# A DeltaNet and MoE kernel: the opening reordered, low weight parts on GpSimd, contiguous sums in the triangular solve

## The reference, cut to what matters

```python
# attention: delta rule, B=4, H=8, S=768, D=48
k_n = k / (norm(k) + 1e-6)
for t in range(S):
    y[t] = q[t] @ state
    state = state + beta[t] * outer(k_n[t], v[t] - k_n[t] @ state)
x = y of all heads, as (3072, 384)
# first expert layer: no nonlinearity between w3 and w_out
x = ((x @ w1) * (x @ w2)) @ w3 @ w_out          # 384 -> 1024 -> 1024 -> 384
# second layer: SoLU, layer norm, projection
h = x @ w_in; s = h * softmax(h); x = layernorm(s) * g @ w_out2
```

## Time and profile before

| | us |
|---|---|
| median of 3 runs (lowest, highest) | 816.47 (814.2, 819.91) |
| the profiled execution | 814.14 |
| its span on the engines | 812.4 |

### The profile page before, as it was taken

One profiled execution on the slowest core, in us unless ns is written; L12 is line 12 of the kernel. 1 busy time (PEld: TensorE's weight loads), 2 busy tenths in 40 slices (PEclk: granted clock), 3 DMA queues, 4 the chain that ended last, 5 costly groups with the idle time before them and its releaser, 6 DMA issues.

```text
span 812.4 us, 22506 instructions
## 1 busy us (share of the span) xinstructions
PE 784.1 (97%) x9708; PEld 711.1 (88%) x9708; DVE 491.3 (60%) x806; ACT 350.0 (43%) x724; POOL 37.5 (5%) x66
## 2 busy tenths in 40 slices
PE   5999899999999999999999999999999999999995
PEld 5557799999999999999999998888889989999894
DVE  1986986696588487759622154443165665656652
ACT  4426235434524633452332344444244454444542
POOL 1100101000100100100000000000010000000000
PEclk9999799999999999999999999999999999999999
DMA  9960332035025014301101575650000000000000
GB/s 288 340 157 8 84 108 78 29 81 144 28 67 157 29 39 116 98 29 41 41 29 42 170 249 162 205 162 1 1 17 23 21 19 22 23 22 19 20 23 26
DMA packets 36552, 65.39 MB, mean 80 GB/s; under 512 B 3184, under 2 KB 25840, under 8 KB 35312
## 3 DMA queue, kind: packets, MB, share of 16 engines
q1 hardware_dynamic: 33888, 58.47, 24.0%
q10 hardware_dynamic: 2576, 5.60, 2.2%
HBM read 45.19 MB, written 18.87 MB: 79 GB/s over the span
## 4 chain that ended last, share of the span: by engine, by line
PE 92%; DMA 3%; DVE 2%; ACT 1%; issue 1%; ACTq 0%; DVEq 0%
PE ps L1326 26%; PE ps L504 12%; PE ps L481 12%; PE ps L468 12%; PE ps L1235 4%; PE ps L1339 4%; PE ps L1259 4%; PE ps L1285 3%; PE ps L1247 3%; PE ps L1287 3%; PE ps L493 2%; DMA mfirst<-in_wo 2%; PE ps L1271 2%; PE ps L1296 2%; DMA m_dram<-msb 1%; PE ps L1310 1%
## 5 line engine op out<-in xcount | busy, mean ns | idle before, releaser
L1141 ACT COPY asb<-ps 128x256 f32<-128x256 f32 x96 | 35.7, 372 | 152.0 <-PE ps L1326 151.3
L950 DVE TENSOR_TENSOR msb<-asb,ps 128x256 f32<-128x256 f32 x96 | 39.9, 416 | 89.9 <-ACT asb L1141 84.7
L504 PE MATMUL ps<-woh,uth 128*128 128x384 f32 x192 | 64.6, 336 | 2.3 <-DVE utl L430 2.3
L504 PE MATMUL ps<-woh,utl 128*128 128x384 f32 x192 | 64.4, 336 | 0.0
L504 PE MATMUL ps<-wol,uth 128*128 128x384 f32 x192 | 64.3, 335 | 0.0
L430 DVE TENSOR_TENSOR utl<-ps,uth 128x512 fp32r<-128x512 f32 x48 | 30.9, 686 | 49.4 <-ACT uth L330 49.4
L1326 PE MATMUL ps<-xh,w1h 128*128 128x256 f32 x288 | 57.7, 310 | 1.9 <-DVE msb L950 1.9
L1235 PE MATMUL ps<-kqs 48*64 48x128 f32 x768 | 48.3, 278 | 10.5 <-DMA kqs<-in_kq 7.4
L316 ACT ACTIVATE e<-ps,stats 128x1024 f32<-128x1024 f32 x24 | 26.8, 1117 | 69.8 <-DVE stats L397 69.8
L468 PE MATMUL ps<-mh,w34h 128*128 128x512 f32 x144 | 56.0, 389 | 0.0
L468 PE MATMUL ps<-ml,w34h 128*128 128x512 f32 x144 | 56.0, 389 | 0.0
(11 more groups left out here) (145 smaller groups left out, 1815.5 us busy)
## 6 DMA issues: line engine op xcount, KB each, us to landing
m_dram<-msb SPq DMA_DIRECT2D x42, 256.0 KB, 2.1
mrest<-m_dram SPq DMA_DIRECT2D x36, 256.0 KB, 6.3
kqs<-in_kq SPq DMA_DIRECT2D x22, 384.0 KB, 7.3
vs<-in_vtok SPq DMA_DIRECT2D x6, 768.0 KB, 9.3
out<-wst SPq DMA_DIRECT2D x24, 192.0 KB
ks<-in_ktok SPq DMA_DIRECT2D x5, 768.0 KB, 5.8
mfirst<-m_dram SPq DMA_DIRECT2D x12, 256.0 KB, 4.1
kqs<-in_w3t SPq DMA_DIRECT2D x4, 512.0 KB, 18.7
```

The costliest lines, as they stand in the source:

```text
L504: ins = pe.matmul(ob, xx[:, j, k, :], w[:, 4 * j + k, :], start=(j == 0 and k == 0 and p == 0), stop=(j == 1 and k == 3 and p == 2))
L950: dve.tensor_tensor(msb[:, f // 2 % 2, f % 2, :], asb[:, f % 2, :], bbank[f % 2], ALU.mult).then_inc(product, 1)
L1141: act.copy(asb[:, f % 2, :], abank[f % 2]).then_inc(a_kept, 1)
```

## The change

It has six pieces.

- **W34.** Only parts 0 to 4 stand ahead of group 0. Parts 5 to 7, 24 steps, are dealt over nine slots of group 0: three steps in each of slots 0 to 5 of `tt` 0, two in slots 6 and 7, and two in slot 0 of `tt` 1.
- **Low parts.** The 16 subtractions `low_w` move from VectorE to GpSimd, after its work on the solve of group 0. ScalarE's first `keep_u` waits for four of them and its first `high_x` for all, since their sources share buffers with `uu` and `ysb`.
- **Squares.** The squares of k for group 0 move from ScalarE to VectorE, and VectorE masks tile 2 ahead of the solve. ScalarE keeps the four Gram tiles in plain order.
- **Solve.** The products of `eights_products` and `second_products` are written with the summed index last, so that the reductions read contiguously. For this they read the second block's inverse transposed: GpSimd writes it into `amat` (`turn_eights`, `turn_sixteen`), and VectorE waits for it (`rows8`, `rows16`). In all groups the eights are joined before slot 7.
- **GpSimd's order.** `scale_v` now also waits for the third step of the solve (the copy L815, after the change L864). `turn_eights` and `turn_sixteen` of each group stand behind that group's `scale_v`.
- **Loads.** k and q of group 0 come in four pieces for each half instead of two. The weights w1 and w2 are loaded ahead of W34's sources 5 to 7, into other buffers. k and q of group 1 are loaded after parts 1 and 3 of W34. v of group 1 still waits for all eight parts.

Lines of the file after the change are about 30 to 40 higher: L1235 is L1272, L1247 is L1284, L1259 is L1296, L1326 is L1363, L1339 is L1376.

```diff
-        first_gbank = [ps[:, b:b + 2, :].rearrange(...) for b in (4, 6, 2, 0)]
+        first_gbank = [ps[:, b:b + 2, :].rearrange(...) for b in (4, 6, 0, 2)]
...
+        FILLS = {(0, 0): 3, (0, 1): 3, (0, 2): 3, (0, 3): 3, (0, 4): 3, (0, 5): 3, (0, 6): 2, (0, 7): 2, (1, 0): 2}
+        FIRST_W34 = KF - 3
...
         def sync(sp):
-            for tt in range(2):
-                sp.dma_start(kqs[0:D, 0, 2 * tt:2 * tt + 2, :, :], kq[0, 0, :, tt]).then_inc(kq_in[0][tt], 16)
+            for tile in range(TPG):
+                sp.dma_start(kqs[0:D, 0, tile:tile + 1, :, :],
+                             kq[0, 0, :, tile // 2, tile % 2:tile % 2 + 1]).then_inc(kq_first[tile], 16)
...
-            for f in range(2, 4):
+            for f in range(2, 5):
                 load_w3(f)
-            for j in range(KF):
+            for j in range(2 * KF):
                 load_w(j)
-            for f in range(4, 6):
-                load_w3(f)
-            for j in range(KF, 2 * KF):
-                load_w(j)
+            load_w3(5)
+            load_k(1)
             for f in range(6, KF):
                 load_w3(f)
-            sp.wait_ge(w34_done, TPG)
-            load_k(1)
+            sp.wait_ge(w34_done, 2)
             load_kq(1, 0)
+            sp.wait_ge(w34_done, 4)
             load_kq(1, 1)
             sp.wait_ge(w34_done, KF)
             load_v(1)
...
         def gpsimd(pool):
                 pool.wait_ge(coef, GCOEF * (n + 1))
+                pool.wait_ge(solve, GSOLVE * n + 3)
...
+            def turn_eights(n):
+                pool.wait_ge(solve, GSOLVE * n + EIGHTS0)
+                pool.sem_inc(pool_passed, 1)
+                pool.tensor_copy(row8(0, [DIAG16, 2], [HB, EB], [1, EB]),
+                                 col8(0, [DIAG16, 2], [1, EB], [HB, EB])).then_inc(rows8, 1)
+
+            def turn_sixteen(n):
+                pool.wait_ge(solve, GSOLVE * n + MERGED8)
+                pool.sem_inc(pool_passed, 1)
+                pool.tensor_copy(amat[:, 0:QB, QB:HB],
+                                 xt[:, QB:HB, QB:HB].rearrange("p j i -> p i j")).then_inc(rows16, 1)
+
+            def low_w(j):
+                pool.wait_ge(w_high, j + 1)
+                pool.sem_inc(pool_passed, 1)
+                pool.tensor_tensor(pieces[j][2], raw[j], pieces[j][1].bitcast(F32), ALU.subtract).then_inc(w_low, 1)
+
             for n in range(NG):
                 scale_v(n)
+                turn_eights(n)
+                turn_sixteen(n)
+                if n == 0:
+                    for j in range(2 * KF):
+                        low_w(j)
...
         def vector(dve):
             def eights_products(n):
                 dve.wait_ge(solve, GSOLVE * n + EIGHTS)
+                dve.wait_ge(rows8, n + 1)
...
             def second_products(n, i0, nj, part):
-                t = tmp[:, 0:QB * EB * nj].rearrange("p (k j i) -> p k j i", k=QB, i=EB)
-                x22 = xt[:, QB:QB + nj, QB + i0:QB + i0 + EB]
+                t = tmp[:, 0:QB * EB * nj].rearrange("p (k i j) -> p k i j", k=QB, i=EB)
                 dve.wait_ge(solve, GSOLVE * n + MERGED8 + 2 * part)
-                dve.tensor_tensor(t, x22.unsqueeze(1).to_broadcast([P, QB, nj, EB]),
-                                  zt[:, :, 0:nj].unsqueeze(3).to_broadcast([P, QB, nj, EB]),
+                dve.wait_ge(rows16, n + 1)
+                dve.tensor_tensor(t, amat[:, i0:i0 + EB, QB:QB + nj].unsqueeze(1).to_broadcast([P, QB, EB, nj]),
+                                  zt[:, :, 0:nj].unsqueeze(2).to_broadcast([P, QB, EB, nj]),
                                   ALU.mult).then_inc(solve, 1)
...
             def second_sums(n, i0, nj, part):
-                dve.tensor_reduce(xt[:, 0:QB, QB + i0:QB + i0 + EB], t.rearrange("p k j i -> p k i j"), AX_X,
+                dve.tensor_reduce(xt[:, 0:QB, QB + i0:QB + i0 + EB], t, AX_X,
                                   ALU.add, negate=True).then_inc(solve, 1)
...
             def group(n, ahead):
-                weights(0, 4)
...
-                weights(4, 6)
...
-                weights(10, 6)
...
-                if ahead and not first:
+                if ahead:
                     eights_first(n + 1)
                 low_x(n, 0, 0)
                 low_x(n, 0, 1)
                 product_of(0, 6)
-                if ahead and not first:
+                if ahead:
                     eights_products(n + 1)
                 product_of(0, 7)

                 right_hand(n, par, 1, 0)
                 right_hand(n, par, 1, 1)
-                if first:
-                    eights_first(n + 1)
-                    eights_products(n + 1)
                 if ahead:
                     eights_sums(n + 1)
```

More of the change, by code:

```diff
@@ L601, in attention_programs @@
         w3_in = [sem(f"w3_in{i}") for i in range(KF)]
+        kq_first = [sem(f"kq_first{i}") for i in range(TPG)]
         kq_in = [[sem(f"kq_in{i}{j}") for j in range(2)] for i in range(2)]
@@ L616, in attention_programs @@
         inverse = sem("inverse")
+        rows8 = sem("rows8")
+        rows16 = sem("rows16")
         ks_done = sem("ks_done")
@@ L649, in attention_programs, with parts @@
         ybank = [ps[:, 2 + g, 0:DM] for g in range(NP)]
+        FILLS = {(0, 0): 3, (0, 1): 3, (0, 2): 3, (0, 3): 3, (0, 4): 3, (0, 5): 3, (0, 6): 2, (0, 7): 2, (1, 0): 2}
+        FIRST_W34 = KF - 3
+        assert sum(FILLS.values()) == 3 * KF
+        def parts(tt, slot):
+            if (tt, slot) not in FILLS:
+                return []
+            at = FIRST_W34 * KF + sum(FILLS[s] for s in FILLS if s < (tt, slot))
+            return [divmod(at + i, KF) for i in range(FILLS[tt, slot])]
         def unit(n, tt, slot):
@@ L677, in attention_programs, with part_of, row8, col8 @@
         MERGED8 = 4 + 2 * (EB - 1) + 7
+        EIGHTS0 = 4 + 2 * (EB - 1)
         GCOEF, GSOLVE = 4, MERGED8 + 8
+        def part_of(mat, first, dims):
+            a = mat[:, :, :]
+            return bass.AP(a.tensor, a.offset + first, [list(a.ap[0]), *[list(d) for d in dims]])
+        def row8(b, *dims):
+            return part_of(amat, b * DIAG16 + EB, dims)
+        def col8(b, *dims):
+            return part_of(xt, b * DIAG16 + DIAG8, dims)
         def sync(sp):
@@ L925, in right_hand2 @@
                 ins.then_inc(rhs2, 1)
-            def low_w(first, count):
-                for j in range(first, first + count):
-                    dve.wait_ge(w_high, j + 1)
-                    dve.tensor_tensor(pieces[j][2], raw[j], pieces[j][1].bitcast(F32),
-                                      ALU.subtract).then_inc(w_low, 1)
             def low_x(n, tt, g):
@@ L955, in group @@
                 par, nxt = n % 2, 1 - n % 2
-                first = n == 0
                 def product_of(tt, slot):
@@ L1098, in keep_u @@
                 act.wait_ge(done, q + 1)
+                if q == 0 and half == 0:
+                    act.wait_ge(w_low, 2 * NP)
                 for bb in range(2):
@@ L1152, in group @@
                     early = ahead and tt == 0
-                    opening = n == 0 and tt == 0
                     def a_of(slot, tt=tt):
@@ L1157, in a_of @@
                             keep_a(*unit(n, tt, slot))
+                        for f, c in parts(tt, slot) if n == 0 else []:
+                            if c == KF - 1:
+                                keep_w34(f)
                     if early:
@@ L1189, in group @@
                     a_of(7)
-            for tt in range(2):
-                act.dma_start(kqs[64:64 + D, 0, 2 * tt:2 * tt + 2, :, :], kq[0, 1, :, tt]).then_inc(kq_in[0][tt], 16)
+            for tile in range(TPG):
+                act.dma_start(kqs[64:64 + D, 0, tile:tile + 1, :, :],
+                              kq[0, 1, :, tile // 2, tile % 2:tile % 2 + 1]).then_inc(kq_first[tile], 16)
             act.dma_start(ks[:, 0, :], ktok[0]).then_inc(k_in[0], 16)
@@ L1352, in fill @@
                         up(half, 1 - tt if slot else tt, f)
-                    elif tt == 0 and 1 <= slot < 5:
-                        w3_wout(KF - 1, range(2 * slot - 2, 2 * slot))
+                    if n == 0:
+                        for f, c in parts(tt, slot):
+                            w3_wout(f, [c])
                 for tt in range(2):
```

73 lines of the change are left out of this document (35 added, 38 removed).

## The result

| | before | after |
|---|---|---|
| median, us (runs) | 814.87 (20) | 819.74 (20) |
| lowest to highest, us | 811.16 to 819.91 | 815.16 to 824.03 |
| the profiled execution, us | 814.14 | 822.29 |
| its span, us | 812.4 | 820.6 |

The ratio is 1.0049, with a 95% interval of 1.003 to 1.0069. The change makes the kernel about half a per cent slower, which is inside 1%.

The account below looks back on a forecast made before the run. TensorE, almost unbroken, with the opening ahead of it, was taken as the bound. The profiled 814.14 us plus 7.2 for the later second chunk gave 821.3; allowing for the median above the profile, 822.5 us, range 817 to 828.

Parts of the forecast that it names:

- Start of the solve: Group 0's transpose after the coefficients, at 20.35 instead of 21.40: -1.05 us (0 to -1.9).
- Contiguous sums: Reductions in group 0's solve, read without a stride: together -3.1 us.
- `scale_v` in the substitution: Group 0's solve: copy gains 2.14 us, substitution product held by `scale_v` loses 2.5 (0 to 2.77); net +0.4.
- Turn copies: `turn_eights` and `turn_sixteen` on GpSimd: 0.7 us beside VectorE, adding 0.1 (0 to 0.7) to group 0's solve.
- Low parts: Subtractions on GpSimd, 0.69 us each, may hold three large products of group 0's solve: +1.0 us (0 to 2.1).
- The rival with 5.5 us: Eight products and sums of the solve each wait for a subtraction, 5.5 us instead of 1.0: 827 us; chance 0.15.
- Sum of the solve: Group 0's solve ends at 51.9 us instead of 54.54, bounds about 49 to 54.5.
- The fall of the clock at the Gram tile: Behind 2.6 us idle at group 1's first Gram tile: 3.4 us at half clock, 1.5 lost (0 to 4.1).
- The wait that decides: TensorE idles 9.8 us behind group 1's late v load; second chunk's `apply_inverse` starts at 98.9, not 91.63: +7.2.
- Spell at half clock behind it: After the second chunk's wait the clock drops as before: costed at nothing, may be up to 2 us shorter.
- Later groups: `scale_v` delays VectorE by 2.5 us, but TensorE loses nothing, by a 0.3 margin; if missed, up to 2 us.
- From the profile to the median: Median shown lies 2.3 us above the profile; forecast put halfway, 822.5 us against 821.3 for the profiled execution.

Follow-up runs that it names:

- e9: e7 with GpSimd's low parts started only after the inverse of group 0 is made; median 806.83 us, ratio 0.9892 to the kernel before.
- e6: e3 with GpSimd's low parts started only after the inverse of group 0 is made; median 803.34 us, ratio 0.9859 to the kernel before.
- e7: e3 with the solve's strided sums as before the change and no turn copies; median 813.14 us, ratio 0.9988 to the kernel before.
- e1: The changed kernel with `turn_eights` ahead of `scale_v` on GpSimd for group 1; median 805.78 us, ratio 0.9878 to the kernel before.
- e3: e1 with six W34 steps instead of three in slot 0 of the first chunk; median 803.66 us, ratio 0.9848 to the kernel before.
- e4: The changed kernel with group 1's products of the eights behind the second chunk's right-hand sides on VectorE; median 815.37 us, ratio 0.9991 to before.

## Why the prediction was right

The mechanism is the forecast one, item by item; two sizes were off, in opposite directions. That part 7 ended within 0.3 us of its forecast is luck: the solve was put 1.3 us too late, and the fall of the clock 1.7 too cheap.

- **Start of the solve.** The transpose into `amat` came at 19.47, not 20.35: -1.93 instead of -1.05, the low bound. k was there at 13.63 instead of 14.32, and the steps behind the squares had no gaps. No run tests the squares or the order of the loads alone.
- **Contiguous sums.** 2.06, 2.00 and 3.85 became 1.28, 1.22 and 2.29: -3.1 as forecast, and e9 shows it again with the sign turned. The Trainium skill, SBUF — State Buffer, section "Door 1: The DMA port swizzle (why [64,N] ≈ [32,N])", says that SBUF is read at full rate only while successive accesses fall into the same 16 bytes, four float32. The old sums stepped by eight float32, the new ones by one: the trace agrees, with sums 1.6 to 1.7 times as long by the larger step.
- **`scale_v` in the substitution.** One product at 2.51 us; held for 2.3 in place of the copy's 2.1. As forecast.
- **Turn copies.** They show 0.8 and 1.6 us, 2.4 together, where 0.7 was taken from the rate of `scale_v`. Most of that is time in which they were held themselves: both began just behind a product of VectorE (28.03 and 33.47) and ended 0.3 and 0.5 us after it. Where VectorE's product had not begun they took 0.4 and 0.6 (last section), 1.0 together. VectorE lost 0.2 by them.
- **Low parts.** 1.00 us each, not 0.69. The joins' products lost 0.7 (e6), where 1.0 was taken. No reduction was held. The rival with 5.5 us fell. That it has a place is shown by e7, where the same subtractions came 9 us earlier and cost 4.6 (38.05 against e9's 33.43): in both, only products were held, and how many depended on when the subtractions ran. The Trainium skill, SBUF — State Buffer, section "Who interferes with whom", adds that the one who comes first keeps the port pair for its whole instruction. The trace agrees: the subtraction at 36.11 took 3.06 us instead of 1.00, since it met a product of 2.33.
- **Sum of the solve.** 50.56 against 51.9. (The bounds of its terms add up to 47.4 to 54.9, not to "about 49 to 54.5".) The first Gram tile started at 51.37 after 1.90 us idle, against 52.7 after 2.6.
- **The fall of the clock at the Gram tile.** It came, but cost 3.2 us instead of 1.5 (bounds 0 to 4.1). This is the term that was mis-sized. Half of the later spell's 3.4 us is already 1.7, and the spell here had 6.8. The loss took back what the early solve had gained, and part 7 was done at 89.4 against 89.1.
- **The wait that decides.** 10.0 against 9.8. The load took 4.9 instead of 4.6, the rest was as listed. `apply_inverse` began at 99.43 against 98.9: +7.8 against +7.2.
- **Spell at half clock behind it.** 8.3 us, the same as before: nothing, as costed.
- **Later groups.** No new waits but 0.4 near 475, as forecast.
- **From the profile to the median.** The profile came to 822.29 (821.3 forecast), the median to 819.74. I had set the median above the profile, since three runs of before lay so. With 20 runs, before has its median 0.7 above its profile, and the changed kernel 2.5 below. Runs differ by their clock: the five shortest of the changed kernel (spans 813.4 to 814.9) had a mean granted clock of 0.988 to 0.992, the five longest (820.1 to 822.3) one of 0.982 to 0.984. As an estimate, 0.004 to 0.010 of 820 us are 3 to 8 us, as much as the spans differ by; run by run the two do not follow each other closely. That a profile with both spells lies in the upper half of its runs is an inference: the other runs have no trace that says which spell they lacked.

## What to carry to other kernels

When an engine takes its list strictly in order, a small instruction that somebody waits for must not stand behind one that waits for a load. Before an operation is put on a lightly used engine, look at what the instruction ahead of it waits for in the worst group, not in the usual one: in groups 2 to 5 this order cost nothing, in group 1 it cost 10 us and the clock. And an edit that takes work away can start other work earlier, as in e7, so look at what its absence releases.

## What the runs showed of the hardware that was not expected

- **Idle time and the clock.** The length of a short idle time alone does not decide whether the clock falls behind it. At the first Gram tile 1.90 us (changed kernel) and 2.32 us (e1) brought a fall; 2.02 us in e9 and 1.46 us before brought none. Ahead of a block of products between 455 and 475, 1.74 us (e7), 1.79 (e1) and 1.80 (e3) brought a fall, while 2.45 in e4 and 1.65 in e6 brought none. And behind the same wait near the end, 1.28 to 1.29 us in all eleven profiles, only e6's clock fell, to 0.50. So one profile doesn't say whether a kernel pays for such an idle time. The two stretches behind e9's Gram tile:

```profile
54.00:58.00 4.00, 3.64 (x97) 1.00 0.01 4
58.00:62.00 4.00, 4.00 (x49) 1.00 0.00 0
```

- **GpSimd is held too, and its rows then look slow.** In groups 2 to 5 of the changed kernel the same turn copies began ahead of VectorE's product and took 0.41 to 0.42 and 0.62 to 0.63 us, though GpSimd had idled for 3 to 7 us. In group 0 they took 0.81 and 1.60, begun 0.15 and 0.13 us behind a product. Held or not decides, and not the waking of the engine. Per element 0.63 us for 256 is 2.5 ns, near the 2.6 of a low part (1.00 us for 384) and above the 1.8 of `scale_v` (2.77 us for 1536). Group 2:

```profile
164.67 0.41 POOL L806 COPY amat<-xt 128x128 f32<-128x128 f32 x1 [3.45 <-DVE xt L879]
...
172.58 0.63 POOL L812 COPY amat<-xt 128x256 f32<-128x256 f32 x1 [7.49 <-DVE xt L911]
```
